# MLP on one core: its first product in fp32 on 32-row quarters of the array, output sums over four banks

## What is computed

```python
def _moe_ref(x, phi, w1, w2):
    ...
    c = logits - logits.max(1, keepdims=True)
    c = np.exp(c)
    c /= c.sum(1, keepdims=True) + 1e-09
    return (c @ slot_out).astype(np.float32)

def _moe2_ref(x, w_in, w_out):
    h = x @ w_in
    g = np.maximum(0.01 * h, h)
    return (g @ w_out).astype(np.float32)
```

## Time and profile before

| | us |
|---|---|
| median of 3 runs | 441.26 (441.08 to 441.61) |
| the profiled execution | 444.33 |
| its span, first to last instruction | 442.5 |
| TensorE busy | 398.4 (90%) |
| VectorE busy | 212.6 (48%) |
| ScalarE busy | 210.3 (48%) |
| GpSimd busy | 11.6 (3%) |
| mean granted clock of TensorE | 0.958 |

### The profile page before, as it was taken

One profiled execution on the slowest core, in us unless ns is written; L12 is line 12 of the kernel. 1 busy time (PEld: TensorE's weight loads), 2 busy tenths in 40 slices (PEclk: granted clock), 3 DMA queues, 4 the chain that ended last, 5 costly groups with the idle time before them and its releaser, 6 DMA issues.

```text
span 442.5 us, 9258 instructions
## 1 busy us (share of the span) xinstructions
PE 398.4 (90%) x3505; PEld 293.2 (66%) x3505; DVE 212.6 (48%) x745; ACT 210.3 (48%) x568; POOL 11.6 (3%) x37
## 2 busy tenths in 40 slices
PE   4886987988897689996799999999999999999997
PEld 3665665766665522332577788888888888888885
DVE  6553344445444343030688854446446446445444
ACT  5665566686675210111889743333334444444331
POOL 2110000000000010000000000000000000000000
PEclk9999899999999569997599999999999999999999
DMA  6878976244232939999940001001001001000101
GB/s 190 310 285 300 348 278 250 86 124 131 86 116 91 398 116 338 386 387 387 386 177 0 1 0 73 0 1 73 0 0 73 0 3 55 16 1 0 73 1 71
DMA packets 25740, 62.08 MB, mean 140 GB/s; under 512 B 1888, under 2 KB 1888, under 8 KB 25696
## 3 DMA queue, kind: packets, MB, share of 16 engines
q1 hardware_dynamic: 22528, 48.91, 30.8%
q0 software_dynamic: 3168, 12.58, 7.9%
HBM read 56.77 MB, written 4.72 MB: 139 GB/s over the span
## 4 chain that ended last, share of the span: by engine, by line
PE 70%; DMA 11%; DVE 8%; ACT 5%; issue 3%; SPq 3%; DVEq 0%; ACTq 0%
PE bank L641 14%; PE bank L642 14%; PE bank L643 14%; DMA kT<-in_k_dram 7%; PE bank L416 5%; PE bank L459 4%; PE bank L448 4%; PE bank L628 3%; DMA ring<-in_moe_w_dram 3%; DVE prob L871 3%; PE bank L469 3%; PE bank L570 3%; DVE x_all L896 2%; PE bank L531 1%; ACT g_stack L790 1%
## 5 line engine op out<-in xcount | busy, mean ns | idle before, releaser
L641 PE MATMUL bank<-w_hi,g_hi 128*128 128x512 f32 x288 | 114.1, 396 | 1.7 <-DVE g_lo L1013 1.7
L643 PE MATMUL bank<-w_hi,g_lo 128*128 128x512 f32 x288 | 113.3, 393 | 0.0
L642 PE MATMUL bank<-w_lo,g_hi 128*128 128x512 f32 x288 | 113.3, 393 | 0.0
L804 ACT COPY h_sb<-bank 128x384 f32<-128x384 f32 x96 | 46.1, 480 | 112.3 <-PE bank L628 112.0
L1006 DVE SCALAR_TENSOR_TENSOR g_sb<-bank,h_sb 128x384 f32<-128x384 f32 x96 | 53.5, 557 | 91.5 <-ACT h_sb L804 91.1
L692 ACT ACTIVATE prob<-prob,row_min 128x192 f32<-128x192 f32 (+1 forms) x144 | 55.7, 430 | 47.4 <-DVE row_min L871 47.3
L641 PEld LDWEIGHTS bank<-w_hi,g_hi 128*128 128x128 f32 x288 | 54.3, 189 | 16.8 <-DVE g_lo L1013 4.6
L643 PEld LDWEIGHTS bank<-w_hi,g_lo 128*128 128x128 f32 x288 | 54.2, 188 | 12.0
L642 PEld LDWEIGHTS bank<-w_lo,g_hi 128*128 128x128 f32 x288 | 54.2, 188 | 8.8
L871 DVE CUSTOM_DVE_ANT_0 prob<-bank,bias 128x192 f32<-128x192 f32 (+1 forms) x144 | 43.9, 324 | 21.6 <-PE bank L416 21.6
L1013 DVE TENSOR_TENSOR g_lo<-g_sb,g_hi 128x384 fp32r<-128x384 f32 x96 | 52.6, 548 | 0.1
(11 more groups left out here) (110 smaller groups left out, 323.8 us busy)
## 6 DMA issues: line engine op xcount, KB each, us to landing
ring<-in_moe_w_dram POOLq DMA_DIRECT2D x6, 2048.0 KB, 11.0
ring<-in_moe_w_dram SPq DMA_DIRECT2D x5, 2048.0 KB, 13.6
ring_late<-in_moe_w_dram SPq DMA_DIRECT2D x3, 2048.0 KB, 10.1
v_one<-in_v_dram SPq DMA_DIRECT2D x16, 325.0 KB, 3.8
qT<-in_q_dram SPq DMA_DIRECT2D x16, 288.0 KB, 4.2
kT<-in_k_dram SPq DMA_DIRECT2D x16, 288.0 KB, 4.7
ring<-in_moe_w_in_dram SPq DMA_DIRECT2D x4, 1024.0 KB, 12.8
ring<-in_moe_w_out_dram SPq DMA_DIRECT2D x8, 512.0 KB, 12.3
```

Source lines behind the costliest of these rows:

```text
L641: nc.tensor.matmul(acc, hi, w_hi[:, f, :], start=(f == 0), stop=False)
L642: nc.tensor.matmul(acc, hi, w_lo[:, f, :], start=False, stop=False)
L643: last = nc.tensor.matmul(acc, lo, w_hi[:, f, :], start=False, stop=(f == FT - 1))
```

## The change

The first product is no longer made from rounded halves. c^T is kept as it is in `cT` (fp32, four times on the partition quarters), G as `project` leaves it in the bank, four blocks on four partition quarters, in `g4`. `ups(qq)` then makes the four first products of four blocks: product j reads the partitions 32j to 32j+31 of both, so it takes 32 rows and all 128 columns of the array, and writes to bank j. The operands are fp32. Banks 0 to 3 now hold h, 4 to 7 the output sums: the sums of all groups are numbered through, and sum `at` lies in bank 4 + at % 4. `project` writes to bank 7. ACT's and DVE's splits of G and DVE's of c go away, with one copy per `project` in their place (`copy_g`); the leaky ReLU reads h_sb only; h_sb and g_sb have four buffers. The lists of TensorE, ACT and DVE in the MLP are written anew. The core of the diff:

```diff
-        c_stack = sb("c_stack", [P, B * S], f32r)
-        g_stack = sb("g_stack", [P, FF], f32r)
+        cT = sb("cT", [P, B * S])
+        g4 = sb("g4", [P, FF // (4 * P), P])
...
-        h_sb = sb("h_sb", [P, 2, GW])
-        g_sb = sb("g_sb", [P, 2, GW])
+        h_sb = ring[:, 4, 0:NR2 * GW].rearrange("p (i n) -> p i n", n=GW)
+        g_sb = sb("g_sb", [P, NR2, GW])
...
                 pe.wait_ge(w_in_loaded[q], 16)
+                if q:
+                    pe.wait_ge(g_copied, q)
...
-                        last = nc.tensor.matmul(bank[3 + q % 3][NS * j:NS * (j + 1), 0:P], soT[:, c, :],
+                        last = nc.tensor.matmul(bank[7][NS * j:NS * (j + 1), 0:P], soT[:, c, :],
...
+            def ups(qq):
+
+                grp, q = divmod(qq, FT // 4)
+                if grp == 0:
+                    pe.wait_ge(g_copied, q + 1)
+                if qq:
+                    pe.wait_ge(h_copied, 4 * qq)
+                for j in range(4):
+                    part = slice(NS * j, NS * (j + 1))
+                    last = nc.tensor.matmul(bank[j][:, 0:GW], g4[part, q, :], cT[part, grp * GW:(grp + 1) * GW],
+                                            start=True, stop=True)
+                last.then_inc(h_done, 1)
+
+            def down(grp, f):
                 kk = grp * FT + f
...
-                    acc = bank[GT * par + t][:, :]
+                    at = GT * grp + t
+                    if f == 0 and at >= 4:
+                        pe.wait_ge(acc_copied, at - 3)
+                    acc = bank[4 + at % 4][:, :]
...
+            pe.wait_ge(soT_copied, 1)
+            project(0)
+            ups(0)
+            for grp in range(NG):
+                for f in range(FT):
+                    down(grp, f)
+                    qq = (grp * FT + f) // 4 + 1
+                    if grp == 0 and f % 4 == 0 and f + 4 < FT:
+                        project(f // 4 + 1)
+                    if f % 4 == 1 and qq < NG * FT // 4:
+                        ups(qq)
+
+
+        def operands_free(eng, kk):
+
+            if kk >= NR2:
+                g0, f0 = divmod(kk - NR2, FT)
                 if f0 == FT - 1:
                     eng.wait_ge(acc_done, GT * (g0 + 1))
...
+            def copy_g(q):
+                act.wait_ge(g_done, q + 1)
+                nc.scalar.copy(g4[:, q, :], bank[7][:, 0:P]).then_inc(g_copied, 1)
+
+            def copy_h(kk):
+                if kk % 4 == 0:
+                    act.wait_ge(h_done, kk // 4 + 1)
+                if kk >= NR2:
+                    act.wait_ge(leaky_done, kk - NR2 + 1)
+                nc.scalar.copy(h_sb[:, kk % NR2, :], bank[kk % 4][:, 0:GW]).then_inc(h_copied, 1)
+
+            def high(kk):
+                act.wait_ge(leaky_done, kk + 1)
+                operands_free(act, kk)
+                nc.scalar.copy(g_hi[:, kk % NR2, :], g_sb[:, kk % NR2, :]).then_inc(ghi_done, 1)
 
             split_w(0)
...
+            copy_g(0)
+            for kk in range(NG * FT):
+                copy_h(kk)
+                if kk % 4:
+                    high(kk - 1)
+                if kk % 4 == 3:
+                    high(kk)
+                if kk % 4 == 1 and kk + 4 < FT:
+                    copy_g(kk // 4 + 1)
+                if kk % 2 == 1 and kk + 1 < FT:
+                    split_w(kk // 2 + 1)
...
+            def leaky(kk):
+                dve.wait_ge(h_copied, kk + 1)
+                if kk >= NR2:
+                    dve.wait_ge(glo_done, kk - NR2 + 1)
+                h = h_sb[:, kk % NR2, :]
+                nc.vector.scalar_tensor_tensor(out=g_sb[:, kk % NR2, :], in0=h, scalar=0.01, in1=h, op0=ALU.mult,
+                                               op1=ALU.max).then_inc(leaky_done, 1)
+
+            def low(kk):
+                dve.wait_ge(ghi_done, kk + 1)
+                operands_free(dve, kk)
+                nc.vector.tensor_tensor(g_lo[:, kk % NR2, :], g_sb[:, kk % NR2, :], g_hi[:, kk % NR2, :].bitcast(f32),
+                                        ALU.subtract).then_inc(glo_done, 1)
 
             split_w(0)
...
+            for kk in range(NG * FT):
+                leaky(kk)
+                if kk % 4:
+                    low(kk - 1)
+                if kk % 4 == 3:
+                    low(kk)
+                if kk % 2 == 1 and kk + 1 < FT:
+                    split_w(kk // 2 + 1)
+                if kk >= FT and kk % FT == 3:
+                    copy_acc(kk // FT - 1)
+            copy_acc(NG - 1)
```

More of the change, by code:

```diff
@@ L613, in project @@
                     for j in range(4):
[L614 removed]
+                        last = nc.tensor.matmul(bank[7][NS * j:NS * (j + 1), 0:P], soT[:, c, :],
                                                 w[:, c, j * P:(j + 1) * P], start=(c == 0), stop=(c == KC - 1))
                 last.then_inc(g_done, 1)
[L618 to L633 removed]
+            def ups(qq):
[10 more added lines that the diff above has]
+            def down(grp, f):
+                kk = grp * FT + f
+                if grp == 0 and f % 2 == 0:
                     pe.wait_ge(w_lo_done, f // 2 + 1)
[L635 to L636 removed]
                 pe.wait_ge(glo_done, kk + 1)
                 for t in range(GT):
[L639 removed]
+                    at = GT * grp + t
+                    if f == 0 and at >= 4:
+                        pe.wait_ge(acc_copied, at - 3)
+                    acc = bank[4 + at % 4][:, :]
                     hi, lo = (x[:, f % NR2, t * P:(t + 1) * P] for x in (g_hi, g_lo))
@@ L784, in _ @@
             nc.scalar.copy(soT[:, :, :].rearrange("p c n -> p (c n)"), bank[5][:, 0:KC * NS]).then_inc(soT_copied, 1)
[L786 to L792, removed]
-            split_w(0)
-            split_g(0)
@@ L796, in _ @@
[L796 to L824, removed]
@@ L991, in split_w, with copy_acc @@
                                         ALU.subtract).then_inc(w_lo_done, 1)
-            def copy_acc(grp, par):
+            def copy_acc(grp):
                 for t in range(GT):
-                    dve.wait_ge(acc_done, GT * grp + t + 1)
-                    if t == 0 and there(grp, 1):
+                    at = GT * grp + t
+                    dve.wait_ge(acc_done, at + 1)
+                    if t == 0 and grp:
                         dve.wait_ge(out_stored, 16 * grp)
-                    nc.vector.tensor_copy(o_sb[:, t, :], bank[GT * par + t][:, :]).then_inc(acc_copied, 1)
@@ L1000, in mlp @@
[L1000 to L1003, removed]
-                    if there(kk, 2):
-                        dve.wait_ge(glo_done, kk - 1)
-                    nc.vector.scalar_tensor_tensor(out=g_sb[:, f % 2, :], in0=bank[6 + f % 2][:, 0:GW], scalar=0.01,
-                                                   in1=h_sb[:, f % 2, :], op0=ALU.mult,
-                                                   op1=ALU.max).then_inc(leaky_done, 1)
-                if there(kk, 1):
-                    lg, lf = (grp, f - 1) if f else (grp - 1, FT - 1)
-                    dve.wait_ge(ghi_done, kk)
-                    operand_waits(dve, lg, lf)
-                    nc.vector.tensor_tensor(g_lo[:, lf % NR2, :], g_sb[:, lf % 2, :],
-                                            g_hi[:, lf % NR2, :].bitcast(f32), ALU.subtract).then_inc(glo_done, 1)
@@ L1016, in groups @@
-            def groups(gg):
-                for par in range(2):
-                    grp = gg * 2 + par
-                    for f in range(FT):
-                        first = known(gg) and gg == 0 and par == 0
-                        if first and f % 2 == 0 and f:
-                            split_w(f // 2)
-                        mlp(grp, par, f)
-                        if first and f + 2 < FT:
-                            split_g(f + 2)
-                        if f == 3 and there(grp, 1):
-                            copy_acc(grp - 1, 1 - par)
```

51 lines of the change are left out of this document (9 added, 42 removed).

## The result

The changed kernel takes 467.87 us (median; 465.37 to 474.63), the kernel before 441.44 in the same comparison: ratio 1.0568, 95% interval 1.048 to 1.0656. One of its four executions, the one of 474.63 us, was in a slow state and is left out of the ratio; the middle one of the other three took 465.57 us. Beside the first experiments it took 469.97 us (ratio 1.0614, 1.0564 to 1.0664). By these ratios the change makes the kernel slower by 25 to 27 us. The profiled execution took 465.37 us.

What follows compares the result with a forecast made beforehand. From 212 us on TensorE was taken as the bound, apart from group 0. Stalls 10.2, clock 4.5, and 5.9 + 6.2 in later groups sum to +26.8 us, put on the median 441.26: 468.1 us, range 456 to 480.

Steps and rivals of the forecast that it cites:

- The fp32 products: In each ups on TensorE: four row-quarter products overlap fully and take 0.65 us.
- the upper bound (2.96): Cost of one ups in us if nothing overlaps, shape change included.
- The change of shape: Around each ups, between full 128x128 products: two changes of array shape cost 0.34 us together.
- The sum for a set of four blocks: One ups at 1.0 us replaces four first products at 0.68 us: +0.32 us per four blocks.
- The rotation over four banks: At five group changes TensorE waits for DVE's copy of a sum: 1.4 us each, 7.0 us in all.
- Group 0: First MLP group: block 0 starts earlier, but copy_g delays high and low after three projects; block 16 +10.2 us.
- The clock: Half clock behind the three stalls of the first MLP group: 1.5 us lost each, +4.5 us.
- the bounds 0 and 7: Lowest and highest total clock loss in us; the highest if half clock lasts as it does up to 219.2 us.
- Groups 1 to 5: Later MLP groups: +5.9 us from 19 ups replacing 77 first products, +6.2 us from stalls at group changes.
- rival 1: Whole MLP: freed ACT and DVE win, block 16 -3.6 us, 436.2 us in all; chance 0.03 faster, 0.02 no change.
- shape priced, no stalls: Case within rival 1: shape changes at 0.34 us for 24 ups, no stall: 8 us more, 444 us.

Runs made afterwards that it cites:

- the first experiments: Changed kernel with project(q+1) ahead of block 4q, with copy_acc ahead of low, and with both edits: 454.44, 461.44 and 448.16 us.
- one full product: Changed kernel, but from the second set on ups is one fp32 product over 128 rows (h incomplete): 459.9 us, ratio 1.0337 to before.
- the copy first: Changed kernel with only DVE's order altered, copy_acc ahead of low(16g+3): 461.44 us, ratio 1.044 to before.
- the last kernel with one full product: Changed kernel with copy_acc ahead of low, copy_g behind high(4q+1), and ups one 128-row product from the second set on: 436.77 us, ratio 0.99.
- the run has 446.3 us: Changed kernel with copy_acc ahead of low and copy_g one block later, behind high(4q+1): 446.29 us, ratio 1.0133 to before.
- the same quarter four times: Changed kernel, but all four products of ups use row quarter 0, each with its own bank: 527.69 us (one execution).

## Why the prediction was right, step by step

- *The fp32 products*, 0.65 us for four with full overlap: 0.65 measured with one full product, four quarters 0.03 us dearer than one. Right, and the upper bound (2.96) is what the products on one quarter cost. The Trainium skill (TensorE: Matmul & The Clock Gate, Measured speedup vs the span model) measured a speedup of 3.07 for four row tiles of 512 columns; by it `ups` would have been an estimated 0.2 us dearer. Here the products on four quarters take 0.86 us to the next second product, the same four on one quarter 2.77: a ratio of 3.2, near the page's, but with the fixed cost of the shape in both. The 0.03 us for three further quarters decide: in the stream the overlap is full.
- *The change of shape*, 0.34 us a pair, from the column quarters of `project`: 0.41 for the row quarters. The mechanism was right and the term 0.07 us too small, 1.6 us in all. The sum for a set of four blocks was +0.32, and 9.24 us (283.95 to 293.19, two L621) less 4 x 2.24 is +0.28, because a term was missing that goes the other way: the forecast kept the second products' steps at 0.230 us, and they fell to 0.227, 36 x 0.003 = 0.1 us. Both small errors nearly cancel.
- *The rotation over four banks*, 1.4 us each: 1.17 of idle, and 1.51 us between sets of four blocks with a group change and without (9.89 and 8.38 us from the L636 behind an `ups` to the next `ups`). Copying first took away 6.8 us. Right by its own chain.
- *Group 0*, +10.2 us of stalls: block 0 started at 6.4 (forecast 6.3); the three waits are 3.53 us each (forecast about 3.8). Block 16 started 14.2 us later than before, 4.2 of them from the clock (below), so 10.0 are left for stalls and shape. The step that mattered was to read ACT's list in its order: a copy that waits for TensorE stands ahead of a cast that TensorE waits for. Moving it alone removed them.
- *The clock*, +4.5, three times 1.5: with the stalls' +10.2 the forecast for block 16 is 64.3, the two executions had 63.8 and 66.0. The size was met, but not in the forecast's way. A half clock followed the stalls two times out of three in the first execution, three out of three in the second, and two out of three in the run with the copy first. In the first execution a block and its `ups` take 3.14 us at full clock (219.97 to 223.11), and 4.70 and 5.73 at the two half clocks (234.07 to 238.77, 249.72 to 255.45), 4.2 us more in all; the second half clock lasted 6.8 us, twice the 3.4 assumed. That two unequal losses come to about three equal ones is luck; the bounds 0 and 7 were needed.
- *Groups 1 to 5*, +12.1: +11.8.
- *Rivals.* The freed helpers did win, but only once the lists were right, and then they made group 0 even with before, no more, with the shape changes and a longer half clock in it. Without the shape changes (the last kernel with one full product) block 16 started 2.4 us earlier than before, of the 3.6 that rival 1 has. Its sum holds two slips that pull against each other: it has five `ups` where four lie between block 0 and block 16 (0.65 us too much), and block 0 at full clock, 2.07 us, where it took 3.71 at the half clock. The forecast for "shape priced, no stalls" was 444 us; the run has 446.3 (445 to 450).
- That the median of 467.9 is met to 0.2 us is chance: the middle one of the three executions in the ratio took 465.6, and the same kernel beside the experiments had 470.0.

What stays open: why the second products' steps are 0.230 us before and 0.227 after. DVE's read of PSUM isn't it. Steps over 0.230 lie behind a first product, where ACT copies its result from a bank, in both kernels; before, that comes four times as often. The two weren't separated. Nor was what the change is worth in the expert stage; it is under what executions differ by ahead of the MLP.

## What to carry to other kernels

Packing small fp32 products on row quarters does make four as cheap as one, but each visit to that shape between full-array products costs 0.4 us here, and the four streams themselves, 0.65 us, save next to nothing against the 0.68 us of the four rounded products they replace. For TensorE's time alone the 0.03 us would need some 14 sets of four in one visit to pay for it, an estimate from these numbers that no run tried; the rest of the gain is the work taken from ACT and DVE. When a list of an in-order engine is rewritten, look at every instruction in it that waits for another engine and at what stands behind it: of the 26 to 28 us, 14 to 16 came from one copy placed a block too early, 7 from another placed a subtraction too late, and both moves cost nothing. The three idle times of 3.5 us of TensorE cost some 40% more in clock (4.2 us on 10.6).

## What the runs showed of the hardware that I had not expected

The clock fell behind products that leave most of the array unused, without any idle time just before: in the run with the same quarter four times TensorE's last idle time, of 1.17 us, ended at 290.31, its records are gapless to 330.4 us (the last 2.84 us of them on one row quarter), and at 330.4 the granted clock was 0.50 for 3.4 us. The same happened at 378.2, 426.0 and 473.8 us, but not behind the 15 other `ups` from block 16 on; why at these is open. In the changed kernel, with 0.93 us on all four quarters, it stayed at 1.00 from 255.8 us to the end, through five idle times of 1.17 us.

A full-array fp32 product of 384 columns costs 0.65 us of the stream, nearly four times the rounded form's 0.17; its two weight loads show no cost beyond that, as 0.65 us is what the forecast had for streaming alone.
